# Pair 2's first FFN: six output steps made into one Strassen product

## What is computed

```
x  = attention(q, mean8(k), mean8(v))          # 2304 x 512
xn = x / sqrt(mean(x*x) + 1e-6) * rms_g
y  = (silu(xn @ w_gate) * (xn @ w_val)) @ w_out   # first FFN:  512 -> 1536 -> 512
z  = silu(y @ w2_in) @ w2_out                     # second FFN: 512 -> 2048 -> 512
```

## Time and profile before

| | |
|---|---|
| median of 3 runs | 884.58 us (884.47 to 885.06) |
| profiled execution, own time | 883.98 us |
| its span in the trace | 882.3 us |
| TensorE busy | 872.0 us, 99%, 4932 matmuls |
| VectorE busy | 504.0 us, 57% |
| ScalarE busy | 342.5 us, 39% |
| GpSimd busy | 266.5 us, 30%, nearly all before 500 us |
| DMA | 191.67 MB, mean 217 GB/s |

### The profile page before, as it was taken

One profiled execution on the slowest core, in us unless ns is written; L12 is line 12 of the kernel. 1 busy time (PEld: TensorE's weight loads), 2 busy tenths in 40 slices (PEclk: granted clock), 3 DMA queues, 4 the chain that ended last, 5 costly groups with the idle time before them and its releaser, 6 DMA issues.

```text
span 882.3 us, 12906 instructions
## 1 busy us (share of the span) xinstructions
PE 872.0 (99%) x4932; PEld 830.3 (94%) x4932; DVE 504.0 (57%) x845; ACT 342.5 (39%) x656; POOL 266.5 (30%) x288
## 2 busy tenths in 40 slices
PE   7999999999999999999999999999999999999998
PEld 6999999999999999998998999999998989989897
DVE  6789757766456666665653346665645444434432
ACT  3679744542222322365552222322233332322222
POOL 6898999882000004567771000000000000000000
PEclk9999999999999999999999999999999999999999
DMA  9971677779755551756778475555545455475321
GB/s 274 269 193 34 264 278 302 286 286 343 289 198 199 204 211 48 280 209 245 292 303 329 179 286 215 215 205 190 205 176 215 179 190 185 166 270 179 131 96 71
DMA packets 55740, 191.67 MB, mean 217 GB/s; under 512 B 21888, under 2 KB 32128, under 8 KB 42624
## 3 DMA queue, kind: packets, MB, share of 16 engines
q1 hardware_dynamic: 55680, 190.85, 60.0%
...
...
## 4 chain that ended last, share of the span: by engine, by line
PE 97%; DVE 1%; DMA 1%; issue 0%; POOL 0%; ACT 0%; SPq 0%; DVEq 0%; POOLq 0%
PE ps L1310 17%; PE ps L1312 16%; PE ps L1311 16%; PE ps L1376 7%; PE ps L1377 7%; PE ps L1375 7%; PE ps L1349 6%; PE ps L1351 6%; PE ps L1350 6%; PE ps L1244 4%; PE ps L1215 2%; PE ps L1227 1%; PE ps L1257 1%; PE ps L1202 1%; DMA kv<-in_k 1%; PE ps L1193 0%
## 5 line engine op out<-in xcount | busy, mean ns | idle before, releaser
L1310 PE MATMUL ps<-xh,wr 128*128 128x384 f32 x840 | 282.4, 336 | 0.1
L1312 PE MATMUL ps<-xh,wr 128*128 128x384 f32 x840 | 281.4, 335 | 0.0
L1311 PE MATMUL ps<-xl,wr 128*128 128x384 f32 x840 | 281.1, 335 | 0.0
L1310 PEld LDWEIGHTS ps<-xh,wr 128*128 128x128 f32 x840 | 157.7, 188 | 2.8 <-DVE qt L1033 1.4
L1311 PEld LDWEIGHTS ps<-xl,wr 128*128 128x128 f32 x840 | 157.8, 188 | 0.9
L1312 PEld LDWEIGHTS ps<-xh,wr 128*128 128x128 f32 x840 | 157.7, 188 | 0.0
L1377 PE MATMUL ps<-wo,al 128*128 128x512 f32 x288 | 112.5, 391 | 0.0
L1376 PE MATMUL ps<-wo,ah 128*128 128x512 f32 x288 | 112.4, 390 | 0.0
L1375 PE MATMUL ps<-wo,ah 128*128 128x512 f32 x288 | 112.0, 389 | 0.0
L1083 DVE TENSOR_TENSOR xacc<-ps,xacc 128x384 f32<-128x384 f32 (+1 forms) x102 | 62.5, 613 | 82.3 <-PE ps L1351 51.5
L794 ACT ACTIVATE ah<-qt 128x384 fp32r<-128x384 f32 x96 | 45.1, 517 | 137.3 <-PE ps L1377 126.2
(11 more groups left out here) (133 smaller groups left out, 1145.4 us busy)
## 6 DMA issues: line engine op xcount, KB each, us to landing
...
```

What stands on the lines that cost most here:

```text
L1310: pe.matmul(out_ps, w_hi, x_hi, start=first and c == 0, stop=False, skip_group_check=True)
L1311: pe.matmul(out_ps, w_hi, x_lo, start=False, stop=False, skip_group_check=True)
L1312: ins = pe.matmul(out_ps, w_lo, x_hi, start=False, stop=c == 1, skip_group_check=True)
```

## The change

Only phase 3 (first FFN of pair 2) computes its output otherwise. Its six output steps are left out. Each group's gated tile goes to a buffer `hid` instead (all 1536 hidden columns of the pair stay in SBUF, where phase 2's forms of x were). After the phase's last unit one `whole` item multiplies them by the whole of `w_out` by the same seven block products: hidden depth in two halves of 768, tokens in two halves of 384, output features in two halves of 256; 7 products x 2 x 6 x 3 = 252 matmuls of 384 columns.

For it the seven forms of `w_out` ("fold": `a` entries are its three raw blocks, `b` entries its four sums, six of each) are made during phases 0 and 1 by ScalarE, GpSimd and SyncE through single buffers `fa` and `fb`, stored to DRAM, and loaded one form a product (three slots) around the whole product. GpSimd and VectorE make the sums of the hidden blocks, ScalarE and VectorE their high and low parts. The forms of x for phase 4 can only be made during the whole product, since phase 3's own stand in the place they need. Units G and V of phase 3, and units 0 and 1 of phase 4, now stand side by side with no output step between. Raw weights of the second FFN's first two units move to other buffers, and in phase 0 the entry `b0` stands ahead of the last output weights (`o` of group 5).

The diff, cut to its core:

```diff
...
     PHASES = [(1, 0), (1, 1), (2, 0), (1, 2), (2, 1), (2, 2)]
+    WHOLE = 3
...
                     items.append(("down", pending))
-            pending = len(downs)
+            pending = None if ph == WHOLE else len(downs)
             downs.append((ph, g))
+        if ph == WHOLE:
+            items.append(("whole", ph))
     items.append(("down", pending))
     NU, ND = len(units), len(downs)
...
+    WPRODUCTS = [(0, 0, 0, True), (2, 3, 3, True), (1, 4, 4, True), (1, 5, 5, False), (0, 1, 1, False),
+                 (1, 2, 6, False), (2, 6, 2, False)]
+    WBANKS = [(0, 2, 3), (4, 5, 6)]
+    PART = 3
+    WLOW_AT = [[], [0, 1, 2], [3, 4], [5], [6, 7], [8, 9], [10]]
+    WHIGH_AT = [[], [0], [1, 2], [3], [4, 5], [6], []]
+    WSUMS = {"u2": 0, "u3": 2, "c22": 3, "c21": 6, "c12": 8}
...
     for g in range(1, GROUPS[1]):
         if g < GROUPS[1] - 1:
             made += [("r", 2 * g + 2), ("r", 2 * g + 3)]
+        if g == GROUPS[1] - 1:
+            made.append(("b", 0))
         made.append(("o", g))
+    FOLD_AT = {}
+    for g in range(5):
+        entries = [("a", 2 * g), ("b", g + 1), ("a", 2 * g + 1)] if g < 3 else [("b", g + 1)]
+        made += entries
+        for what, entry in zip(("gate", "down", "value") if g < 3 else ("down",), entries):
+            FOLD_AT[what, g] = entry
     U2, N2 = first_unit[2], last_down[1] + 1
     made += [("r", U2), ("r", U2 + 1), ("o", N2)]
     for i in range(GROUPS[2] - 1):
...
+        if kind == "a":
+            return 7 + x % 2
         ph, letter, g, _ = units[x]
         if letter == "I":
-            return g if g < 2 else 3
+            return (2, 0)[g] if g < 2 else 3
         return 0 if letter == "G" else 1
...
+        hid = at(x_at[0], "hid", [P, 4, 2 * PART, BLOCK])
...
+        def gated_home(n, c):
+            if classic[n]:
+                return vt[:, c, :]
+            g = downs[n][1]
+            return hid[:, 2 * (g // PART) + c % 2, 2 * (g % PART) + c // 2, :]
...
-                if raw_next[i] is not None:
+                if raw_next[i] is not None and made[raw_next[i]] != ("r", U2 + 1):
                     load_raw(raw_next[i])
                 sp.wait_ge(s_wlo, i + 1)
-                if kind == "r":
+                if kind in "ab":
+                    lo, hi = (0, 3) if kind == "a" else (3, NF)
+                    sp.dma_start(f_dram[lo:hi, :, 2 * FF * x:2 * FF * (x + 1)].rearrange("f p n -> p f n"),
+                                 fold_bits[kind]).then_inc(s_ast if kind == "a" else s_bst, 16)
+                elif kind == "r":
                     sp.dma_start(r_dram[r_home(x), :, :], wr_bits[x % RING][:, :])\
...
+            def load_fold(i):
+                if i == 0:
+                    sp.wait_ge(s_ast, 16 * 2 * PART)
+                    sp.wait_ge(s_bst, 16 * 2 * PART)
+                    sp.wait_ge(s_down, down0[first_group])
+                elif i < 3:
+                    sp.wait_ge(s_prod, NF * (last_unit[WHOLE] + i - 1))
+                else:
+                    sp.wait_ge(s_wh, 2 * (i - 2))
+                sp.dma_start(fw_bits[i % 3][:, :], f_dram[WPRODUCTS[i][1], :, :]).then_inc(s_fw[i % 3], 16)
             def load_out(n):
                 sp.wait_ge(s_down, down0[o_before(n) + 1])
...
+                if item == ("unit", 10):
+                    keep(made_at["b", 0])
+                if item == ("unit", 12):
+                    load_raw(made_at["a", 0])
+                    load_raw(made_at["a", 1])
+                if kind == "down" and ("gate", x - last_down[0]) in FOLD_AT:
+                    keep(made_at[FOLD_AT["gate", x - last_down[0]]])
+                if kind == "unit" and units[x][0:2] == (1, "V"):
+                    for what in ("down", "value"):
+                        if (what, units[x][2]) in FOLD_AT:
+                            keep(made_at[FOLD_AT[what, units[x][2]]])
+                    if units[x][2] == 4:
+                        load_raw(made_at["r", U2 + 1])
+                if item == ("unit", last_unit[WHOLE] - 2):
+                    load_fold(0)
+                if item == ("unit", last_unit[WHOLE]):
+                    load_fold(1)
+                if kind == "whole":
+                    for i in range(2, NF):
+                        load_fold(i)
...
+            def fold_sums(i):
+                r = raw[raw_of(i)][:, :].rearrange("p (k n) -> p k n", k=2)
+                a11, a12, a21, a22 = r[:, 0, 0:FF], r[:, 1, 0:FF], r[:, 0, FF:2 * FF], r[:, 1, FF:2 * FF]
+                s1, s2, s3, s4 = [fbt[:, f, 1, :] for f in range(4)]
+                if made[i] == ("b", 0):
+                    pool.wait_ge(s_wlo, made_at["r", last_unit[0]] + 1)
+                else:
+                    pool.wait_ge(s_bst, 16 * made[i][1])
+                pool.wait_ge(s_raw[raw_of(i)], 16 * raw_count[i])
+                pool.tensor_tensor(s1, a21, a22, ALU.add).then_inc(s_ws, 1)
+                pool.tensor_tensor(s3, a11, a21, ALU.subtract)
+                pool.wait_ge(s_ws, sums0[i] + 1)
+                pool.tensor_tensor(s2, s1, a11, ALU.subtract).then_inc(s_ws, 1)
+                pool.wait_ge(s_ws, sums0[i] + 2)
+                pool.tensor_tensor(s4, a12, s2, ALU.subtract).then_inc(s_ws, 1)
+            def fold_low(i):
+                r = raw[raw_of(i)][:, :].rearrange("p (k n) -> p k n", k=2)
+                pool.wait_ge(s_whi, his0[i + 1])
+                if made[i][0] == "a":
+                    pool.tensor_tensor(fa[:, 0:2, 1, :], r[:, :, 0:FF], fa[:, 0:2, 0, :], ALU.subtract)
+                    pool.tensor_tensor(fa[:, 2, 1, :], r[:, 1, FF:2 * FF], fa[:, 2, 0, :], ALU.subtract)\
+                        .then_inc(s_wlo, 1)
...
+            def hidden_sums(f, j):
+                b11, b12, b21, b22 = [hid[:, i, 2 * j:2 * j + 2, :] for i in range(4)]
+                if f == 3:
+                    pool.wait_ge(s_flo, j + 1)
+                    pool.wait_ge(s_hd, hd0[first_group + j + 1])
+                    pool.tensor_tensor(b11, b12, b11, ALU.subtract).then_inc(s_ft, 1)
+                elif f == 5:
+                    pool.wait_ge(s_ft, j + 1)
+                    pool.wait_ge(s_hd, hd0[first_group + PART + j + 1])
+                    pool.tensor_tensor(b12, b22, b12, ALU.subtract).then_inc(s_ft, 1)
+                else:
+                    pool.wait_ge(s_flo, 2 * PART + j + 1)
+                    pool.tensor_tensor(b11, b21, b11, ALU.subtract).then_inc(s_ft, 1)
...
+                if kind == "a":
+                    r = raw[raw_of(i)][:, :].rearrange("p (k n) -> p k n", k=2)
+                    if x:
+                        act.wait_ge(s_ast, 16 * x)
+                    else:
+                        act.wait_ge(s_prod, NF * (last_unit[0] + 1))
+                    act.activation(fa[:, 0:2, 0, :], r[:, :, 0:FF], ACT.Copy).then_inc(s_whi, 1)
+                    act.activation(fa[:, 2, 0, :], r[:, 1, FF:2 * FF], ACT.Copy).then_inc(s_whi, 1)
+                    return
+                if kind == "b":
+                    act.wait_ge(s_ws, sums0[i + 1])
+                    act.activation(fb[:, :, 0, :], fbt[:, :, 1, :], ACT.Copy).then_inc(s_whi, 1)
                     return
...
+            def form_high(i):
+                f = WPRODUCTS[i][2]
+                for j in range(PART):
+                    if i == 0:
+                        act.wait_ge(s_hd, hd0[downs.index((WHOLE, j)) + 1])
+                        act.wait_ge(s_down, down0[downs.index((WHOLE, 0))])
+                    elif i == 1:
+                        act.wait_ge(s_hd, hd0[downs.index((WHOLE + 1, 0))])
+                        act.wait_ge(s_wlo, len(made))
+                    else:
+                        act.wait_ge(s_wh, 2 * (i - 1))
+                    if f in (3, 5, 6):
+                        act.wait_ge(s_ft, (3, 5, 6).index(f) * PART + j + 1)
+                    elif f == 4:
+                        act.wait_ge(s_ft2, j + 1)
+                    act.activation(fh[i % 2][j][:, :, :], hidden_part(f, j), ACT.Copy).then_inc(s_fhi, 1)
...
+            def act_whole():
+                for i in range(NF):
+                    if i + 1 < NF:
+                        form_high(i + 1)
+                    if i == 0:
+                        whole_copy(0, 0)
+                        whole_copy(0, 1)
+                    if i == 5:
+                        whole_copy(4, 0)
+                        whole_copy(4, 1)
+                    for f in WHIGH_AT[i]:
+                        token_high(WHOLE + 1, f)
...
             def act_unit(x):
                 ph, letter, g, n = units[x]
-                prior = ffn_of[n - 1] if n and letter != "V" else None
-                if before["unit", x] == ("unit", 0):
-                    silu(0, 2)
-                    silu(0, 3)
+                prior = ffn_of[n - 1] if n and letter != "V" and classic[n - 1] else None
+                if before["unit", x] and before["unit", x][0] == "unit" and units[before["unit", x][1]][1] != "V":
```

(88 more changed lines are left out.)

234 lines of the change are left out of this document (185 added, 49 removed).

## The result

| | median | runs | against before |
|---|---|---|---|
| before | 884.53 us | 884.36 to 885.06 (4) | |
| changed | 897.84 us | 896.33 to 899.02 (4) | 1.0149 [1.0131, 1.0166] |
| predicted | 890.3 us | range 882.5 to 896.0 | 1.0065 |

The account below looks back on a forecast made before the run. TensorE, busy 99% of the span, was taken as the bound: matmul count times spacing, plus few holes. Terms -6.25 + 4.5 + 7.5 = +5.75 us took the median from 884.58 to 890.3 us, range 882.5 to 896.

Parts of the forecast that it names:

- The matmuls removed: Pair 2's first FFN: 252 matmuls replace 288, 36 fewer at 0.1736 us on TensorE, -6.25 us.
- (a): Unit V4, phase 3: VectorE's three low parts behind G4 delay the fourth product, 1.2 us, bounds 1.0 and 2.4.
- (d): Phase 4's units I0 and I1 side by side: ScalarE's queued work delays I1's first copy and addition, 1.3 us.
- (c): Inside the whole product: VectorE's first addition beside GpSimd's sums, which the fourth product awaits, 0.3 us, bounds 0 and 1.5.
- The late sum: Costs added from phase 3 to phase 4, four terms together: +4.5 us, bounds stated as 3.9 and 6.6.
- (b): Start of the whole product: it waits bare for gates 0 to 2 of V5, 1.7 us.
- rival 3: Whole product: VectorE becomes the bound as GpSimd's sums collide with its work, 3 us more, 893 us; chance 0.07.
- The early part: Phases 0 and 1: folded-weight jobs waiting for transfers hold ScalarE's copies for TensorE, +7.5 us, bounds 3 and 13.
- the backlog: Phase 1, groups 0 to 2: 389 GB/s needed over 378, so a3 and a5 late once each, 1.0 us (0 to 4).
- Rival 2: Phase 1's first three groups: the DMA queue is the bound, 2.4 us per group late, 896.5 us; chance 0.12.
- Rival 1: Phases 0 and 1: the queue keeps up, early part costs 0 to 1 us, 882.5 us; chance 0.20.
- Rival 4: Phases 0 and 1: half the early cost, only u12 and next pair's V0 wait, 885.8 us; chance 0.08.

Follow-up runs that it names:

- experiment 10: Changed kernel with b0 behind o5, a0 and a1 loaded first, b3 to b5 set apart, and three late edits: 881.96 us, ratio 0.9969.
- experiment 7: Changed kernel with the whole product's first block waiting only for its own bank, the first gate of unit V5: 897.62 us.
- experiment 6: Changed kernel with the seventh form's three sums made by VectorE during the fourth product, not by GpSimd: 892.07 us.
- experiment 4: Changed kernel with b0 behind o5, a0 and a1 loaded first, and b3, b4, b5 moved to G3, G4, V4: 890.46 us.

## Why the prediction was wrong

**The matmuls removed, -6.25.** Right: 4932 - 4896 = 36, and in experiment 10 they are what makes the kernel faster. The late stage adds up: -6.25 + 2.4 + 1.6 + 2.9 + 1.25 for the holes of (a) to (d), + 3.0 for the clock behind two of them, + 0.4 for four restarts = +5.3, as measured.

**What was left out: the clock behind a hole.** The prediction priced a hole at its length and 0.1 for the restart. That holds for holes up to 2.1 us. Three holes of the profiled run were longer and cost 1.5 us more each, 4.5 us of the 7.5 by which the forecast missed; most of the rest are the collisions in (c), 2.6, and (a), 1.2. This is the largest failed step, and the kernel before could not have shown it, having no hole of that length past its attention part.

**(a) Low parts of form 0 behind G4, 1.2 taken, 1.0 to 2.4 the bounds.** The hole is 2.56, its cost 2.4, with the clock 3.9. VectorE's three took 4.31 and GpSimd's three 6.75. The step that failed is the choice of half a microsecond a collision, taken from the one 1.47 at 188.58. The GpSimd operation in its way was not the one of the earlier trace rows but the one before that, and it had only 0.65 us left to run when VectorE's began (the one of the earlier trace rows in turn took 2.03 because it came behind VectorE's):

```profile
187.92 1.31 POOL L600 TENSOR_TENSOR wr<-wt,wr 128x512 fp32r<-128x512 f32 x1
```

So the row showed the remainder of one operation, not the price of a collision; here GpSimd's sums last 1.85 and follow one another. The upper bound was nearly exact. It was the one that the Trainium skill's rule gave (SBUF — State Buffer, "SBUF: two separate sides": the two engines share a port pair under an exclusive lock, and the loser is blocked for the whole of it). This case's runs agree with the rule: 0.95 became 2.49, and 0.55 became 1.49. (The late sum's bounds were also added wrongly: the terms as given make 4.0 and 6.9, not 3.9 and 6.6.)

**(b) The start of the whole product, 1.7.** The hole is 1.79, a cost of 1.6. The size is right, but it is not a cost of its own: taken away, it came back whole at the fourth product (experiment 7).

**(c) Inside the whole product, 0.3, bounds 0 and 1.5.** The hole is 3.11, a cost of 2.9, with the clock 4.4. This is rival 3's mechanism, and experiment 6 shows it. The chain that I worked out put the first addition at 18.4 after V5's end against 20.4 due. It was built on uncontended durations and left 2 us for collisions; the collisions took 4.8 (1.54 and 3.29) in the two rows at 608.84 and 611.25 alone. Rival 3 priced it at 3 us and 7%; its reason there, a VectorE with too much to do, was wrong too, since with three sums more it was on time.

**(d) I0 and I1 side by side, 1.3.** The hole is 1.42, a cost of 1.25 in every one of the kernels. Right.

**The early part, +7.5.** Measured 8.8, of which 1.5 is the clock behind unit 13's hole; the holes' own 7.1 are near the forecast. Its parts, by the lag of each unit's first addition: u11 1.7 (0.6 taken), u12 1.9 (1.3), u13 3.4 (3.2), a1 none (1.4), a3 and a5 none (1.0). The sum was right by luck, because errors cancelled. b0's raw landed at 214.98, but the sums ended only at 218.8, one of them 1.45 in place of 0.74 beside VectorE: the lock again. a0 landed at 245.48, later than the 242.4 taken, and its unit was itself later. What was overpriced is the backlog. At a share of 1.00 to 1.02 the queues moved more than the 378 GB/s on which I had built it:

```profile
260.00:270.00 10.00, 10.00 (x59) 10.00 (x58) 4.88 (x10) 3.63 (x7) 5.81 (x7) 1.00 1.02 397
...
290.00:300.00 10.00, 10.00 (x60) 10.00 (x59) 6.88 (x9) 3.73 (x7) 4.72 (x4) 1.00 1.01 418
```

So no step was late past 258 us. The Trainium skill's 358 GB/s between HBM and a core (SBUF — State Buffer, "A bandwidth-pool intuition that's wrong") is further off: the trace has 397 and 418, and the measurement decides.

**The rivals.** Rival 2 (896.5, bandwidth) comes nearest in time and is wrong in mechanism: in experiments 4 and 10 the same bytes pass with an early lag of 0.9 and 1.5. What cost the time was which work stood in front of which: on ScalarE's queue, in the rooms `raw_c` and `fb`, and, for a0, in the DMA queue. Rival 1 (882.5, the early cost falls away) did not happen, but experiment 4 shows its price well enough, 7.4 us. Rival 4 (half of the early cost) did not happen either.

What stays open: why the clock fell behind some holes of the same length and not behind others (next section but one).
